# Spectral FFN on one Trainium2 core: low halves of the inverse-transform rows by TensorE and ScalarE from the third tile on, and another order of VectorE's spectral steps

## The chip, the cores and the metric

The kernel runs on one core of one Trainium2 chip. The metric is the device time of one execution in microseconds (us), the lower the better. The engines are TensorE (PE; its weight loads are PEld), VectorE (DVE), ScalarE (ACT), GpSimd (POOL) and SyncE (SP), each with its own instruction stream in program order; they meet through semaphores.

## What is computed

The reference has two parts in a row. The first is a spectral layer over x of shape 4 x 3008 x 256:

```
X  = rfft(x, axis=1)
Yr = Xr @ w_r - Xi @ w_i + b_r ;  Yi = Xr @ w_i + Xi @ w_r + b_i
Yr, Yi = sign(Y) * max(|Y| - 0.01, 0)
y  = irfft(Yr + i Yi, n=3008, axis=1)
```

The second is a feed-forward layer over all 12032 rows of y: h = y @ w_in (256 to 2048), g = (a0 + a1 h + a2 h^2 + a3 h^3) / (1 + |b0||h| + |b1| h^2 + 1e-6), out = g @ w_out (2048 to 256).

## The kernel before

The transform is factored as 3008 = 47 x 64. Step 1 (`step_s1`, 64 of them) transforms along one factor; its result goes to DRAM (`spec1`). Steps 2, 3 and 4 (`step_s2`, `step_s3`, `step_s4`, 96 of each: 24 in each of four batches) do the other factor, the mix with w_r and w_i with the threshold, and the inverse of that factor; the result goes to DRAM (`spec2`). Step 5 (`step_s5`) is the last part of the inverse and gives the rows of the feed-forward layer, transposed.

The feed-forward layer runs over 26 tiles (numbered from 0) of 470 rows (the last has 282). Each tile has 8 slots, so there are 208 slots; a slot handles 256 of the 2048 hidden columns. In a slot q the engines do, for a full tile:

- PE: `group_f2_hi(q-3)`, 8 matmuls; `group_f2_lo(q-3)`, 4 matmuls; `group_f1(q+2)`, 12 matmuls in float16; then spectral steps that fall into the slot, in the order 4, 3, 2, 1, 5 (lines 648 to 700).
- ACT: evacuations of steps 2, 1 and 5, then `group(q+1)` (three activations, den, sq, num, with the `below` of step 3 ahead of num), the store buffer o_sb once in a tile, a reciprocal root (L846), a square (L849), and the evacuation of step 4 (L750).
- DVE: L1087 and L1090 of slot q, `multiplied(q-2)` (L1067), `rounded(q-1)` (L1062), `remainder(q-2)` (L1073), and spectral steps between them: `lower_x` (L945, L948), `soft` (L954), `measure_x`, `measure`, `coefficients`, and `split_lo` (L1022).
- POOL: g_lo of group q-3 (L1148), which needs `remainder`, then a DMA that adds sq into den for group q+1 (L1140).

Step 2 is done in slots 0, 2, 4 and so on up to 138, without 94, 112 and 130; its step 3 comes one slot later and its step 4 three slots later. Step 1 is in slots 0 to 30 and 40 to 70, even ones. Step 5 of tile t is done in halves in slots 8(t-1)+1 and 8(t-1)+3 (`S5_AT`), so halves of tiles 2 to 18 are in slots 9 and 11, 17 and 19, up to 137 and 139. The steps 2, 4 and 5 share one PSUM bank, d0; 1 and 3 share d1. The waits that keep the shared bank in order are on the counts e4, e2l, e5l and k_top.

Every row tile is kept as two float16 parts, yt_hi and yt_lo, and `group_f1` multiplies both. There are two ways in which yt_lo is made:

- Tiles below 19: ACT evacuates the half of step 5 with the tile's scale into yt_hi (L762), and DVE's `split_lo` reads the bank again and writes bank x scale - yt_hi to yt_lo (L1022).
- Tiles from 19 on (`LATE_TILES`): step 5 uses a matrix that has the scale in it (`c5_scaled`, two of them, written by DVE at L1104 in slot 142). ACT copies the bank into yt_hi (L759) in the slot after; PE then adds -yt_hi to the bank with one matmul (`rest_of_s5`, L538) at the end of that slot; ACT copies the bank to yt_lo (L768) at the start of the slot after that.

`measure_x` is in slots 34 and 76, and `measure` with `coefficients` in slots 40, 88 and 142 (one set of scales for each combination of batches in a tile, seven in all; the first is made ahead of slot 0).

Of the kernel before, what the change touches and what calls it, by code (L numbers as in the profile page):

```python
# [19 lines left out]
ROWS = NJ * N2P  # L20
# [144 lines left out]
LATE_TILES = range(ENTRY[-1], NT)  # L165
# [19 lines left out]
def spectral_ffn(nc, x, c1, c5, fwd, inv, w_r, w_i, bias, w_in, w_out, coef_a, coef_b, out):  # L185
    with ExitStack() as ctx:
# [38 lines left out]
        c5_scaled = several("c5_scaled", 2, ROWS, PC)  # L225
# [69 lines left out]
        def scaled_c5(t):  # L295
            return c5_scaled[set_of(t) - set_of(LATE_TILES[0])]

# [158 lines left out]
        def _(pe):  # L456
# [64 lines left out]
            def step_s5(idx, bank):  # L521
                t, half = divmod(idx, KH)
                later = t in LATE_TILES
                pe.wait_ge(s_zp[t % 2], zp_count[t])
                if later:
                    pe.wait_ge(k_c5, set_of(t) - set_of(LATE_TILES[0]) + 1)
# [126 lines left out]
            for q in range(NS + 2):  # L653
# [6 lines left out]
                if q == NS + 1:  # L660
                    group_f2_lo(NS - 2)
                    group_f2_lo(NS - 1)
                if q + 2 < NS:
                    group_f1(q + 2)
# [34 lines left out]
                if q - 1 in S5_AT and S5_AT[q - 1] // KH in LATE_TILES:  # L699
                    rest_of_s5(S5_AT[q - 1], d0[:, :])  # L700

        @block.scalar
        def _(act):
# [49 lines left out]
            def evacuate_s5(idx, bank):  # L753
# [4 lines left out]
                if t in LATE_TILES:  # L758
# [6 lines left out]
            def evacuate_rest(idx, bank):  # L765
                t, half = divmod(idx, KH)
                act.wait_ge(e5r, idx - KH * LATE_TILES[0] + 1)
                act.activation(yt_lo[t % 2][:, half, 0:tile_cols(t)], bank[:, 0:tile_cols(t)], ACT.Copy).then_inc(e5l, 1)  # L768

            def group(q, c=None):  # L770
# [9 lines left out]
                if c is not None:  # L780
                    below(c, d1)
                act.activation(ring(num, q), h, ACT.Identity, bias=scales(q // SLOTS, 4),  # L782
                               scale=scales(q // SLOTS, 5)).then_inc(n_num, 1)

# [33 lines left out]
            for q in range(NS + 2):  # L818
# [11 lines left out]
                if q - 2 in S5_AT and S5_AT[q - 2] // KH in LATE_TILES:  # L830
                    evacuate_rest(S5_AT[q - 2], d0[:, :])
                if 1 <= q < NS - 1:
                    group(q + 1, S2_AT.get(q - 2))
# [22 lines left out]
        def _(dve):  # L856
# [149 lines left out]

            def weight_lo(i):
# [24 lines left out]
            for u in range(1, PRE + 1):  # L1032
# [16 lines left out]
                if u == K2 + 2:  # L1049
                    measure(0, (d0, d1)[(u - 1) % 2])  # L1050
                    coefficients(0)
                if u == PRE - 1:
# [30 lines left out]
            for q in range(NS + 2):  # L1083
# [8 lines left out]
                if q == 0:  # L1092
                    lower_x(PRE, d0[:, :])
                if q - 1 in S2_AT and q >= 2:
                    lower_x(S2_AT[q - 1], d0[:, :])
                if q - 1 in Y_AT:
                    n = Y_AT.index(q - 1)
                    measure(n, d0)
                    for i in range(len(SETS)):
                        if SETS[i][-1] == n:  # L1100
                            coefficients(i)
                        if SETS[i][-1] == n == B - 1:
                            dve.wait_ge(s_ff, 16)
                            dve.tensor_scalar(c5_scaled[i - set_of(LATE_TILES[0])][:, :], c5_sb[:, :],  # L1104
                                              coef[0:ROWS, i, 0:1], None, ALU.mult).then_inc(k_c5, 1)
                if 0 <= q - 2 < NS and late(q - 2):
                    multiplied(q - 2)
                if 0 <= q - 1 < NS:
# [3 lines left out]
                if q - 1 in S5_AT and S5_AT[q - 1] // KH not in LATE_TILES:  # L1112
# [66 lines left out]
```

## Time and profile before

| | us |
|---|---|
| median of 3 runs (lowest, highest) | 1448.93 (1446.75, 1450.62) |
| the profiled execution | 1448.17 |
| its span, first to last instruction | 1445.9 |
| PE busy | 1393.1 (96%) |
| DVE busy | 1324.2 (92%) |
| ACT busy | 1252.1 (87%) |
| POOL busy | 630.4 (44%) |

The granted clock of TensorE is 0.99 of full over the span. Around the span lie 2.3 us. Busy time counts neighbours that overlap in the pipeline once, and matmul ends are modelled, so a PE that is busy without a gap is seen better from the starts of its instructions than from their lengths. The slots run from 128 us (start of DVE's slot 0) to the end.

### The profile page before, as it was taken

The numbers are of one execution on the slowest core, as the hardware profiler recorded it, in microseconds if no ns is written. First come the engines' busy times: TensorE is split into PE (matmuls) and PEld (weight loads), VectorE is DVE, ScalarE is ACT, GpSimd is POOL, SyncE is SP. The second block draws the span as 40 slices with busy tenths as digits, with TensorE's granted clock in tenths as the row PEclk, the third lists the DMA queues.
The fourth block names the chain that finished last, engine by engine and source line by source line (L and its number), as shares of the span: only waits on it lengthen the run. The fifth ranks groups of instructions, "written<-read, shape, count | busy, mean of one in ns | idle before, by whom it ended". The sixth has DMA issues, their size and how long they took to land.

```text
span 1445.9 us, 21576 instructions
## 1 busy us (share of the span) xinstructions
PE 1393.1 (96%) x7498; PEld 972.8 (67%) x7498; DVE 1324.2 (92%) x1650; ACT 1252.1 (87%) x1657; POOL 630.4 (44%) x417
## 2 busy tenths in 40 slices
PE   7998999999999999999999999999989999999987
PEld 2876766667667676776766676776766666666666
DVE  5676989989999889899999999999999999999998
ACT  3577989988989989889879988988988999999986
POOL 0000444444444444444445445544545555555554
PEclk8999999999999999999999999999999999999999
DMA  8885665666556655555555545555545555555443
GB/s 257 265 258 137 151 152 136 143 144 137 108 124 150 142 119 134 136 114 118 110 120 114 126 108 123 124 113 111 114 105 108 107 94 110 118 108 110 86 97 70
DMA packets 97913, 188.07 MB, mean 130 GB/s; under 512 B 11216, under 2 KB 57744, under 8 KB 97808
## 3 DMA queue, kind: packets, MB, share of 16 engines
q0 software_dynamic: 29952, 98.58, 36.8%
q1 hardware_dynamic: 67856, 88.12, 20.7%
q8 instruction: 62, 1.02, 0.3%
q14 instruction: 43, 0.35, 0.1%
HBM read 50.60 MB, written 37.49 MB: 61 GB/s over the span
## 4 chain that ended last, share of the span: by engine, by line
PE 52%; DVE 20%; ACT 16%; issue 8%; DMA 2%; POOL 2%; SPq 0%; ACTq 0%; DVEq 0%; POOLq 0%
PE h_ps L552 18%; PE o_ps L582 7%; PE o_ps L567 6%; PE o_ps L569 6%; DVE num L1073 4%; DVE den L1067 4%; DVE g_hi L1062 4%; DVE num L1087 4%; PE d L529 3%; ACT sq L779 3%; ACT den L776 3%; ACT num L782 3%; ACT sq L846 3%; PE d L493 2%; POOL g_lo L1148 2%
## 5 line engine op out<-in xcount | busy, mean ns | idle before, releaser
L1148 POOL TENSOR_TENSOR g_lo<-num,sq 128x940 fp32r<-128x940 f32 (+1 forms) x205 | 453.1, 2210 | 153.2 <-DVE num L1073 153.1
L1140 POOL DMA_DIRECT2D den<-sq x208 | 182.5, 877 | 649.6 <-ACT sq L779 345.4
L567 PE MATMUL o_ps<-g_hi,wout_hi 128*128 128x470 f32 (+1 forms) x832 | 342.0, 412 | 1.0 <-DVE g_hi L1062 1.0
L569 PE MATMUL o_ps<-g_hi,wout_lo 128*128 128x470 f32 (+1 forms) x832 | 310.3, 374 | 0.0
L552 PE MATMUL h_ps<-yt_hi,win_hi 128*128 128x470 f16 (+1 forms) x832 | 302.2, 363 | 3.7 <-DVE num L1090 3.7
L552 PE MATMUL h_ps<-yt_hi,win_lo 128*128 128x470 f16 (+1 forms) x832 | 300.1, 361 | 0.0
L552 PE MATMUL h_ps<-yt_lo,win_hi 128*128 128x470 f16 (+1 forms) x832 | 300.0, 361 | 0.0
L1090 DVE SCALAR_TENSOR_TENSOR num<-num,coef,h_ps 128x940 f32<-128x940 f32 (+1 forms) x208 | 245.2, 1179 | 7.4
L1073 DVE SCALAR_TENSOR_TENSOR num<-num,a_sb,den 128x940 f32<-128x940 f32 (+1 forms) x208 | 244.6, 1176 | 0.1
L1062 DVE SCALAR_TENSOR_TENSOR g_hi<-num,a_sb,sq 128x940 fp32r<-128x940 f32 (+1 forms) x208 | 244.5, 1175 | 0.0
L779 ACT ACTIVATE sq<-h_ps,coef 128x940 f32<-128x940 f32 (+1 forms) x208 | 214.6, 1032 | 32.1 <-POOL g_lo L1148 31.9
L582 PE MATMUL o_ps<-g_lo,wout_hi 128*128 128x470 f32 (+1 forms) x832 | 216.0, 382 | 25.8 <-POOL g_lo L1148 24.9
L1087 DVE TENSOR_TENSOR num<-h_ps,num 128x940 f32<-128x940 f32 (+1 forms) x208 | 231.7, 1114 | 9.9 <-ACT num L782 9.6
L1067 DVE SCALAR_TENSOR_TENSOR den<-den,g_hi 128x940 f32<-128x940 f32 (+1 forms) x208 | 238.9, 1148 | 0.1
L782 ACT ACTIVATE num<-h_ps,coef 128x940 f32<-128x940 f32 (+1 forms) x208 | 234.2, 1126 | 0.0
L846 ACT ACTIVATE sq<-den,qone 128x940 f32<-128x940 f32 (+1 forms) x208 | 223.7, 1075 | 3.4 <-DMA den<-sq 3.4
L776 ACT ACTIVATE den<-h_ps,coef 128x940 f32<-128x940 f32 (+1 forms) x208 | 213.0, 1024 | 6.5 <-DVE num L1073 4.3
L849 ACT ACTIVATE sq<-sq 128x940 f32<-128x940 f32 (+1 forms) x208 | 203.2, 977 | 6.6
L582 PEld LDWEIGHTS o_ps<-g_lo,wout_hi 128*128 128x128 f32 x832 | 151.4, 190 | 64.0 <-POOL g_lo L1148 46.1
L567 PEld LDWEIGHTS o_ps<-g_hi,wout_hi 128*128 128x128 f32 x832 | 157.8, 190 | 31.0 <-issue 8.3
L569 PEld LDWEIGHTS o_ps<-g_hi,wout_lo 128*128 128x128 f32 x832 | 158.0, 190 | 23.4 <-issue 7.5
L552 PEld LDWEIGHTS h_ps<-yt_hi,win_hi 128*128 128x128 f16 x832 | 81.3, 98 | 113.9 <-issue 48.7
(161 smaller groups left out, 1576.8 us busy)
## 6 DMA issues: line engine op xcount, KB each, us to landing
den<-sq POOLq DMA_DIRECT2D x200, 470.0 KB, 4.4
spec<-s1w SPq DMA_DIRECT2D x64, 192.0 KB, 2.7
z_in<-spec SPq DMA_DIRECT2D x96, 128.0 KB, 2.5
spec<-s_out SPq DMA_DIRECT2D x96, 128.0 KB, 1.9
xw<-in_x SPq DMA_DIRECT2D x31, 384.0 KB, 4.7
out_t<-o_sb SPq DMA_DIRECT2D x25, 470.0 KB, 4.0
zp_in<-spec SPq DMA_DIRECT2D x22, 480.0 KB, 5.3
inv_in<-in_inv SPq DMA_DIRECT2D x96, 64.0 KB, 2.2
```

What stands on the lines that cost most here:

```text
L552: mm = pe.matmul(h_ps[q % 2][:, j, 0:cols(q)], w[:, h, f * P:(f + 1) * P], y[t % 2][:, h, 0:cols(q)], start=i == 0, stop=i == len(terms) - 1)
L567: pe.matmul(o_ps[:, h, 0:w], wout_hi[:, f, h * P:(h + 1) * P], g_hi[q % 3][:, j, 0:w], start=f == 0, stop=False)
L569: mm = pe.matmul(o_ps[:, h, 0:w], wout_lo[:, f, h * P:(h + 1) * P], g_hi[q % 3][:, j, 0:w], start=False, stop=False)
L582: mm = pe.matmul(o_ps[:, h, 0:w], wout_hi[:, f, h * P:(h + 1) * P], g_lo[q % 2][:, j, 0:w], start=False, stop=f == FB - 1)
L779: act.activation(ring(sq, q), h, ACT.Square, scale=scales(q // SLOTS, 3)).then_inc(n_sq, 1)
L782: act.activation(ring(num, q), h, ACT.Identity, bias=scales(q // SLOTS, 4), scale=scales(q // SLOTS, 5)).then_inc(n_num, 1)
L846: act.activation(ring(sq, q), ring(den, q), ACT.Abs_reciprocal_sqrt, bias=qone[:, 0:1]).then_inc(n_rs, 1)
L1062: dve.scalar_tensor_tensor(out=g_hi[r % 3][:, :, 0:w], in0=ring(num, r), scalar=a_sb[:, 0:1], in1=ring(sq, r), op0=ALU.add, op1=ALU.mult). ...
L1067: dve.scalar_tensor_tensor(out=ring(den, r), in0=ring(den, r), scalar=1.0 + 1e-6, in1=g_hi[r % 3][:, :, 0:cols(r)].bitcast(F32), op0=ALU.a ...
L1073: dve.scalar_tensor_tensor(out=ring(num, r), in0=ring(num, r), scalar=a_sb[:, 0:1], in1=ring(den, r), op0=ALU.add, op1=ALU.subtract).then_ ...
L1087: dve.tensor_tensor(top, h, top, ALU.mult).then_inc(n_n2, 1)
L1148: pool.tensor_tensor(g_lo[r % 2][:, :, 0:cols(r)], ring(num, r), ring(sq, r), ALU.mult).then_inc(n_g, 1)
```

## The change

Four things change.

1. `LATE_TILES` (19 to 25) becomes `PE_TILES` (2 to 25). `c5_scaled` has seven buffers, one for each set, and DVE writes the one that belongs to a set right behind that set's `coefficients`.
2. PE issues `rest_of_s5` in the same slot, but behind `group_f2_lo(q-3)` and ahead of `group_f1(q+2)`, no longer at the slot's end.
3. ACT copies the bank to yt_lo (`evacuate_rest`) in that same slot, behind the num activation of `group(q+1)`, no longer at the start of the next slot.
4. On DVE `lower_x` stands behind `multiplied(q-2)`, no longer ahead of `measure`; `remainder(q-2)` stands ahead of `soft` and `measure_x`, no longer behind them.

```diff
-LATE_TILES = range(ENTRY[-1], NT)
+PE_TILES = range(2, NT)
...
-        c5_scaled = several("c5_scaled", 2, ROWS, PC)
+        c5_scaled = several("c5_scaled", len(SETS), ROWS, PC)
...
+                if q - 1 in S5_AT and S5_AT[q - 1] // KH in PE_TILES:
+                    rest_of_s5(S5_AT[q - 1], d0[:, :])
                 if q + 2 < NS:
                     group_f1(q + 2)
...
                 if q in S5_AT:
                     step_s5(S5_AT[q], d0[:, :])
-                if q - 1 in S5_AT and S5_AT[q - 1] // KH in LATE_TILES:
-                    rest_of_s5(S5_AT[q - 1], d0[:, :])
...
                 act.activation(ring(num, q), h, ACT.Identity, bias=scales(q // SLOTS, 4),
                                scale=scales(q // SLOTS, 5)).then_inc(n_num, 1)
+                if rest is not None:
+                    evacuate_rest(rest, d0[:, :])
...
-                if q - 2 in S5_AT and S5_AT[q - 2] // KH in LATE_TILES:
-                    evacuate_rest(S5_AT[q - 2], d0[:, :])
                 if 1 <= q < NS - 1:
-                    group(q + 1, S2_AT.get(q - 2))
+                    group(q + 1, S2_AT.get(q - 2), S5_AT[q - 1] if S5_AT.get(q - 1, 0) // KH in PE_TILES else None)
...
+            def scaled_matrix(i):
+                dve.wait_ge(s_ff, 16)
+                dve.tensor_scalar(c5_scaled[i][:, :], c5_sb[:, :], coef[0:ROWS, i, 0:1], None, ALU.mult).then_inc(k_c5, 1)
...
-                if q == 0:
-                    lower_x(PRE, d0[:, :])
-                if q - 1 in S2_AT and q >= 2:
-                    lower_x(S2_AT[q - 1], d0[:, :])
                 if q - 1 in Y_AT:
                     n = Y_AT.index(q - 1)
                     measure(n, d0)
                     for i in range(len(SETS)):
                         if SETS[i][-1] == n:
                             coefficients(i)
-                        if SETS[i][-1] == n == B - 1:
-                            dve.wait_ge(s_ff, 16)
-                            dve.tensor_scalar(c5_scaled[i - set_of(LATE_TILES[0])][:, :], c5_sb[:, :],
-                                              coef[0:ROWS, i, 0:1], None, ALU.mult).then_inc(k_c5, 1)
+                            scaled_matrix(i)
                 if 0 <= q - 2 < NS and late(q - 2):
                     multiplied(q - 2)
+                if q == 0:
+                    lower_x(PRE, d0[:, :])
+                if q - 1 in S2_AT and q >= 2:
+                    lower_x(S2_AT[q - 1], d0[:, :])
                 if 0 <= q - 1 < NS:
                     rounded(q - 1)
                 if 1 <= q <= KH:
                     split_lo(KH + q - 1, o_ps[:, q - 1, :])
-                if q - 1 in S5_AT and S5_AT[q - 1] // KH not in LATE_TILES:
+                if q - 1 in S5_AT and S5_AT[q - 1] // KH not in PE_TILES:
                     split_lo(S5_AT[q - 1], d0[:, :])
+                if 0 <= q - 2 < NS and late(q - 2):
+                    remainder(q - 2)
+                    if on_vector(q - 2):
+                        lower(q - 2)
                 if q - 2 in S2_AT:
                     soft(S2_AT[q - 2], d1)
...
-                if 0 <= q - 2 < NS and late(q - 2):
-                    remainder(q - 2)
-                    if on_vector(q - 2):
-                        lower(q - 2)
```

## Rows read from the trace of the kernel before

**Rows 1.** The page, part 1: busy time, share, instructions of each engine.

```profile
PE 1393.1 (96%) x7498; PEld 972.8 (67%) x7498; DVE 1324.2 (92%) x1650; ACT 1252.1 (87%) x1657; POOL 630.4 (44%) x417
```

**Rows 2.** Busy time by stretch (start:end, length, then each engine's).

```profile
247.71:262.57 14.86, 14.38 (x82) 10.11 (x80) 11.76 (x15) 13.45 (x19) 5.58 (x4) 1.00 0.42 90
262.57:303.12 40.55, 40.55 (x218) 28.53 (x219) 38.30 (x45) 37.00 (x52) 19.02 (x13) 1.00 0.72 159
357.70:372.65 14.95, 13.71 (x80) 9.86 (x79) 13.11 (x25) 12.56 (x16) 5.25 (x5) 1.00 0.41 85
945.50:959.28 13.78, 13.57 (x79) 9.67 (x77) 12.29 (x16) 12.38 (x16) 5.67 (x5) 1.00 0.39 82
1150.56:1195.21 44.65, 43.42 (x215) 28.93 (x214) 44.31 (x41) 41.99 (x46) 24.76 (x16) 1.00 0.54 109
```

**Rows 3.** Waits of the whole span: waiter, releaser, us, times, longest.

```profile
PEld d L529 <- ACT s_out L750: 11.1, 16, 1.7
```

**Rows 4.** Timeline, slots 18 and 19: start, length, instruction, idle before it.

```profile
247.71 1.25 PE L529 MATMUL d<-c_sb,zp_in 96*128 96x94 f32 x10
249.00 0.65 ACT L762 ACTIVATE yt_hi<-d,coef 128x470 f16<-128x470 f32 x1 [2.03 <-PE d L529]
...
251.85 1.15 ACT L782 ACTIVATE num<-h_ps,coef 128x940 f32<-128x940 f32 x1
...
253.78 0.61 PE L469 MATMUL d<-fwd_sb,z_in 128*128 128x128 f32 x4
...
262.06 0.46 ACT L750 ACTIVATE s_out<-d,x_inv 128x256 f32<-128x256 f32 x1
262.57 1.35 PE L529 MATMUL d<-c_sb,zp_in 96*128 96x94 f32 x10 [0.48 <-ACT s_out L750]
```

**Rows 5.** Instruction groups by shape: count, busy us, mean ns, idle before.

```profile
L1022 DVE SCALAR_TENSOR_TENSOR yt_lo<-d,coef,yt_hi 128x470 f16<-128x470 f32 x34 | 23.8, 701 | 2.3 <-ACT yt_hi L762 2.3
L1104 DVE TENSOR_SCALAR c_scaled<-c_sb,coef 96x94 f32<-96x94 f32 x2 | 0.5, 268 | 0.1
```

**Rows 6.** Timeline of ACT in slots 154 and 155, a late tile.

```profile
1191.22 0.56 ACT L759 ACTIVATE yt_hi<-d 128x470 f16<-128x470 f32 x1 [0.61 <-PE d L529]
...
1197.42 0.54 ACT L768 ACTIVATE yt_lo<-d 128x470 f16<-128x470 f32 x1
1197.86 1.04 ACT L776 ACTIVATE den<-h_ps,coef 128x940 f32<-128x940 f32 x1
```

**Rows 7.** Timeline of PE's weight loads around the late tile's extra matmul.

```profile
1195.82 0.10 PEld L538 LDWEIGHTS d<-yt_hi,minus_one 128*128 128x128 f16 x1
1196.02 0.19 PEld L567 LDWEIGHTS o_ps<-g_hi,wout_hi 128*128 128x128 f32 x1
```

**Rows 8.** The chain that ended last: start, length, what; one group_f1.

```profile
149.00 2.40 PE h_ps L552 x12
```

**Rows 9.** Timeline, slot 34, and PE behind it.

```profile
362.14 0.88 POOL L1140 DMA_DIRECT2D den<-sq  x1 [4.41 <-PE o_ps L582]
...
363.90 1.20 DVE L1073 SCALAR_TENSOR_TENSOR num<-num,a_sb,den 128x940 f32<-128x940 f32 x1
...
367.44 1.13 PE L582 MATMUL o_ps<-g_lo,wout_hi 128*128 128x470 f32 x4 [1.24 <-POOL g_lo L1148]
```

**Rows 10.** Timeline, slots 84, 88 and 142, and PE behind slot 76.

```profile
657.52 1.13 PE L582 MATMUL o_ps<-g_lo,wout_hi 128*128 128x470 f32 x4 [1.26 <-POOL g_lo L1148]
...
705.20 1.15 ACT L782 ACTIVATE num<-h_ps,coef 128x940 f32<-128x940 f32 x1
705.36 0.42 DVE L954 SCALAR_TENSOR_TENSOR ythr<-d,neg 128x256 f32<-128x256 f32 x1 [0.61 <-ACT neg L739]
...
706.82 1.13 DVE L1087 TENSOR_TENSOR num<-h_ps,num 128x940 f32<-128x940 f32 x1
...
736.62 1.12 PE L582 MATMUL o_ps<-g_lo,wout_hi 128*128 128x470 f32 x4 [2.26 <-POOL g_lo L1148]
...
1084.76 1.93 PE L582 MATMUL o_ps<-g_lo,wout_hi 128*128 128x470 f32 x4 [3.54 <-POOL g_lo L1148]
```

More of the change, by code:

```diff
@@ L295, in scaled_c5 @@
         def scaled_c5(t):
-            return c5_scaled[set_of(t) - set_of(LATE_TILES[0])]
+            return c5_scaled[set_of(t)]
         def cols(q):
@@ L522, in step_s5 @@
                 t, half = divmod(idx, KH)
-                later = t in LATE_TILES
+                later = t in PE_TILES
                 pe.wait_ge(s_zp[t % 2], zp_count[t])
                 if later:
-                    pe.wait_ge(k_c5, set_of(t) - set_of(LATE_TILES[0]) + 1)
+                    pe.wait_ge(k_c5, set_of(t) + 1)
                 matrix = scaled_c5(t) if later else c5_sb
@@ L757, in evacuate_s5 @@
                     act.wait_ge(f1, (t - 1) * SLOTS)
-                if t in LATE_TILES:
+                if t in PE_TILES:
                     act.activation(yt_hi[t % 2][:, half, 0:tile_cols(t)], bank[:, 0:tile_cols(t)], ACT.Copy).then_inc(e5, 1)
@@ L766, in evacuate_rest, with group @@
                 t, half = divmod(idx, KH)
-                act.wait_ge(e5r, idx - KH * LATE_TILES[0] + 1)
+                act.wait_ge(e5r, idx - KH * PE_TILES[0] + 1)
                 act.activation(yt_lo[t % 2][:, half, 0:tile_cols(t)], bank[:, 0:tile_cols(t)], ACT.Copy).then_inc(e5l, 1)
-            def group(q, c=None):
+            def group(q, c=None, rest=None):
                 h = h_ps[q % 2][:, :, 0:cols(q)]
@@ L1051, in _ @@
                     coefficients(0)
+                    scaled_matrix(0)
                 if u == PRE - 1:
```

## The prediction

> **What bounds the kernel now.** I read the page's shares first. PE is busy for 96% of the span, DVE 92%, ACT 87% [rows 1]: three engines are near full, so shares alone don't tell what a microsecond on each is worth. The view by stretch does. While spectral steps run (slots 3 to 141, tiles 0 to 17), cut a tile's 8 slots at the two halves of step 5. From the second half to the next tile's first, PE is busy for 40.55 of 40.55 us while DVE works 38.30 and ACT 37.00 [rows 2]: PE sets the pace. Between the two halves it isn't quite so: 14.86 us, PE 14.38, and the stretch ends with PE waiting for ACT's evacuation of step 4 [rows 2, 4]. The timeline of ACT there has no gap: released by step 5 at 249.00, it runs through to 262.52, and step 5's other half starts at 262.57 [rows 4]. So this stretch is a loop through ACT's queue. The same wait stands in the list of waits 16 times [rows 3]; I count it in all 17 tiles but two. The exceptions are slot 35, where PE is late for another reason (below), and slot 115, which has no step 4; the sixteenth is the first half in slot 113. From slot 142 on, DVE is the bound: 44.31 busy of 44.65 us, PE 43.42 [rows 2].
>
> So VectorE, which the change relieves, is the bound in the last third only, where nothing is taken from it.
>
> **Part 1: split_lo leaves DVE.** 34 instructions of 0.70 us, 23.8 us in all [rows 5]. By the stretches above they lie beside PE's or ACT's work: worth nothing by themselves, but for the places in part 4.
>
> **Part 2: 34 more matmuls on PE.** In a late tile the same matmul's weight load starts at 1195.82 and the next one's at 1196.02, so it takes 0.20 us of PE's queue [rows 7]; 12 float16 matmuls of group_f1 take 2.40, again 0.20 each [rows 8]. The matmul now stands between float32 and float16 ones, which no row shows: bounds 0.10 (the transition partly hides it) and 0.30; I take 0.20, the spacing of its own kind. Its wait is over in time: yt_hi is done about 1.9 us after step 5 began (249.00 + 0.65 against 247.71) [rows 4], while PE still has the rest of step 5 and 12 matmuls of group_f2 in between, over 2.4 us at the spacing just named. Queued behind it are group_f1 and steps 4 to 1.
>
> The Trainium skill, "TensorE: Matmul & The Clock Gate", section "Back-to-back issue gap", gives a sustained 131 ns for a matmul of 512 columns in a stream of weight loads and matmuls. The trace differs, 0.20 us at 470 columns [rows 8]; by the page's figure part 2 would be about 4.5 us in place of 6.8, before anything is hidden, an estimate.
>
> **Part 3: 34 more copies on ACT.** One takes 0.54 us, but the next instruction starts 0.44 after it [rows 6]. The copy to yt_hi becomes one without a scale operand, 0.56 instead of 0.65 [rows 4, 6], 0.09 less. Net 0.35 in each slot that has one. The copy stands behind num, so DVE's L1087 isn't delayed; o_sb, the root and the square are, and with them the end of the ACT loop.
>
> Who waits for it: step 2 in the same slot, by the count e5l, since the bank is shared. num ends at 253.0 now (251.85 + 1.15), in future 0.09 earlier; the copy behind it ends by 253.45, while PE reaches step 2 at 253.78, in future 0.20 later [rows 4]. Cover about 0.5 us. If that cover were gone, each 0.1 us beyond would cost 34 x 0.1 = 3.4 us.
>
> The Trainium skill, "ScalarE: Activation LUTs", section "Rules for kernel authors", says to use VectorE, not ScalarE, for simple arithmetic; it speaks against this move. For this operation the trace has DVE at 0.70 and ACT at 0.54 [rows 5, 6]: per instruction it differs from the rule. By the rule the copy would take 0.70 or more, 0.16 x 15 = 2.4 us on top of the sum, an estimate.
>
> **Part 4: the order on DVE.** remainder goes ahead of soft and measure_x. Where that counts:
> - Slot 34: remainder starts at 363.90, behind the soft's wait and nine small instructions; PE then waits 1.24 us for the g_lo behind it, released by POOL [rows 9], and has taken some 0.16 more in the matmul before, 1.40 in all. With the new order remainder is some 3 us earlier, and POOL can start when its DMA ends, at 363.02 [rows 9], so 2.1 us before 365.1, where remainder ends now. The wait goes whole. Slot 76 is alike, 1.26 us [rows 10], 1.42 in all.
> - Slots 84 to 88: DVE runs without a gap from slot 84, where it has a wait of 0.61 and the split_lo, up to the coefficients in slot 88, behind which PE waits 2.26 us [rows 10]. With both gone, what is late next is ACT's num: 705.20 + 1.15 = 706.35, less 0.09, against L1087 at 706.82 now [rows 10]. Gain about 0.5; the two new c5_scaled cost 2 x 0.18 of queue (0.27 us long) [rows 5], which soft's move behind remainder (0.35) takes back. The same 0.5 in front of slot 142, behind which PE waits 3.54 and which leads into the stage that DVE bounds [rows 10]. In slot 40 step 1 waits for soft, which now comes later: +0.1.
> - lower_x behind multiplied: a slot's group_f1 (2.40 us) [rows 8] stands ahead of its reader, step 3, on PE. Nothing.
> - Elsewhere PE doesn't wait for DVE or POOL, so nothing.
>
> **The sum**, per stretch.
> - First to second half, 15 tiles bound by ACT: +0.35 each (PE's 0.20 fits under it), 5.25. Slot 115's: +0.20. Slots 33 to 35: the stretch is 14.95 now; the stall goes, and next is the ACT loop, 13.78 where there is no step 1 [rows 2], plus 0.35, 14.13: -0.8. Together +4.65.
> - Second half to next tile, 17: 11 at +0.20 are 2.2; slot 40 +0.1; slot 76 -1.42 + 0.20 = -1.2; slot 88 -0.5; slot 142 -0.5; two around the slots that have no step 2 (94, 112), where PE loses a few tenths to POOL, -0.5 together, an estimate from those slots' pace. Together -0.4.
> - From slot 142 on: the copy only moves within ACT's queue, DVE's work is the same: 0. Ahead of slot 3 one c5_scaled more (0.27 us) under a wait for ACT: 0.
>
> Sum +4.2 us on the profiled execution's 1448.2, 1452.4. That one is 0.8 below the median of the runs; from the median it would be 1453.1. I say 1452.8.
>
> **The rivals.**
> - A, the gains don't come: POOL or ACT holds slots 34, 76, 88, 142 as DVE did. For: POOL's DMA stands in the way in slot 34. Against: it ends in time. 17 x 0.35 + 17 x 0.20 = +9.4: 1458.
> - B, slower by one mechanism: step 2 waits for the yt_lo copy on the shared bank. Place: slots 10, 12, 18, 20 and so on. It decides once ACT's copy ends over 0.5 us later than I place it. At 0.2 beyond, 34 x 0.2 = 6.8 on top of 4.2: 1460. For: ACT's queue there is without gaps. Against: both sides hang on the same step 5, so the cover is the same in each tile.
> - C, the matmul is cheap (0.10) and PE's small losses to DVE and POOL go with DVE's relief: 11 x 0.10 less and some 2 us from 8 tiles without step 1: 1449.5.
> - D, faster: the bound in tiles 9 to 17 is really DVE, which works 38.30 of 40.55 us in such a stretch [rows 2]. Then 1.2 us of split_lo goes in each of 9 tiles, 10.8, against 2 of additions: 1440. Against: PE has no idle time in that stretch [rows 2].
> - E, the change doesn't do what it says (split_lo stays, the matmul goes elsewhere): the code leaves no room for it.
>
> **How the numbers follow.** Forecast (1450.5 to 1455) 0.50, C 0.22, A 0.12, B 0.07, D 0.09. 0.3% of 1448.9 is 4.3 us, about what a measurement can tell from no change: 1444.6 to 1453.3. Of the forecast's chance 0.28 lies below 1453.3, so same = 0.28 + 0.22 = 0.50; faster is D, 0.09; slower 0.22 + 0.12 + 0.07 = 0.41. The range reaches from 1446.5, below C (the added matmuls at 0.10 throughout, and all waits of PE for POOL gone), to 1458, A; outside are D and B. Its ends follow the two unknown costs: 34 matmuls at 0.10 or 0.30, and the copy at 0.44 or 0.54.
>
> **What would show it.** In the profile after: L1022 down to 4 instructions; DVE's busy time down by 20 or more us and the span not; the stretch from step 5 to step 5 at 15.2 us with step 1 and 14.1 without, ended by ACT's s_out; the other stretch at 40.75 with PE busy throughout; no PE wait for POOL behind slots 34 and 76; DVE idle where it worked. The prediction is wrong if the first stretch doesn't grow (then ACT's queue wasn't the loop), if the other shrinks (then PE wasn't the bound), or if step 2 starts late behind L768.

## The result, and the profile after

The changed kernel takes 1453.35 us (median; 1450.94 to 1455.58), the kernel before 1448.39 (1446.71 to 1450.62) on the same chip. The ratio is 1.0033 with a 95% interval of 1.0023 to 1.0042: slower by about 5 us. I had said 1452.8; by my own bounds for no change, 0.3%, the time lies just above the edge. The profiled execution took 1452.47 with a span of 1450.5 against 1445.9 (4.5 more; both are rounded).

First the page's busy times. They answer to [rows 1]:

```profile
PE 1394.7 (96%) x7532; PEld 976.5 (67%) x7532; DVE 1315.8 (91%) x1621; ACT 1262.1 (87%) x1691; POOL 631.9 (44%) x417
```

PE and ACT have their 34 instructions more, DVE has 29 fewer. DVE's busy time fell by 8.4 us only. The groups of instructions by shape say why:

```profile
L768 ACT ACTIVATE yt_lo<-d 128x470 f16<-128x470 f32 x46 | 26.8, 583 | 0.0
L1009 DVE TENSOR_SCALAR c_scaled<-c_sb,coef 96x94 f32<-96x94 f32 x7 | 1.9, 267 | 0.2
L1072 DVE SCALAR_TENSOR_TENSOR den<-den,g_hi 128x940 f32<-128x940 f32 x200 | 237.5, 1188 | 0.0
L1150 POOL TENSOR_TENSOR g_lo<-num,sq 128x940 fp32r<-128x940 f32 x200 | 462.9, 2315 | 89.4 <-DVE num L1078 89.2
```

23.8 us of split_lo went [rows 5] and 1.4 of c5_scaled came. But `multiplied` (L1072) now has a mean of 1188 ns and 237.5 us in all, where L1067 had 231.5 before, and POOL's g_lo has 2315 ns where L1148 had 2227: the same work shows as longer, on both engines. For POOL that goes with what stands in front: its g_lo lasts 2.16 to 2.23 us wherever POOL stood idle before it (172 of 200 before, 117 now), and 2.4 to 2.5 in most cases where it follows POOL's DMA instruction at once (13 times before, 79 now). Why, no row shows. POOL's waits for `remainder` fell from 153.1 us to 89.2, most of which shortened nothing.

`multiplied` is held by POOL. Two lines of slot 18:

```profile
245.58 2.50 POOL L1150 TENSOR_TENSOR g_lo<-num,sq 128x940 fp32r<-128x940 f32 x1
247.76 1.32 DVE L1072 SCALAR_TENSOR_TENSOR den<-den,g_hi 128x940 f32<-128x940 f32 x1
```

g_lo ends at 248.08, `multiplied` 1.00 later. So it is each time: of the 200 full ones 150 take 1.13 us, and none of them starts more than 0.14 ahead of g_lo's end; the other 50 start 0.29 to 1.04 ahead of it and end 1.00 after it (0.99 to 1.01). In the kernel before there are 26 of those. Over 1.13 they make up 11.5 us in place of 5.5, which is the 6.0.

The span is read better by stretch. The same columns as in [rows 2], same stretches in the changed kernel, in time order:

```profile
248.58:263.80 15.22, 14.57 (x83) 10.20 (x81) 11.78 (x15) 13.81 (x20) 5.99 (x4) 1.00 0.41 89
263.80:304.46 40.66, 40.66 (x218) 28.60 (x219) 37.72 (x43) 37.30 (x53) 18.74 (x13) 1.00 0.69 157
359.65:373.90 14.25, 13.77 (x81) 9.95 (x80) 12.18 (x22) 12.74 (x17) 4.27 (x4) 1.00 0.37 78
949.84:963.98 14.14, 13.70 (x80) 9.85 (x78) 12.72 (x16) 12.74 (x17) 6.44 (x5) 1.00 0.39 80
```

From first to second half of step 5 it is 15.22 for 14.86, and 14.14 for 13.78: +0.36 each. From second half to the next tile it is 40.66; from start of step 5 to start of step 5 it had been 40.49 (the row in [rows 2] ends 0.06 later), so +0.17.

Cutting the whole span at the starts of step 5 and adding up (us, after less before):

| stretches | foretold | measured |
|---|---|---|
| first to second half, 15 bound by ACT | +5.25 | +5.40 |
| the one from slot 113 | +0.20 | +0.17 |
| slots 33 to 35 | -0.8 | -0.70 |
| second half to next tile, 11 of 17 | +2.2 | +1.75 |
| from slot 35 (slot 40) | +0.1 | +0.28 |
| from slot 75 (slot 76) | -1.2 | -0.17 |
| from slot 83 (slot 88) | -0.5 | -0.50 |
| from slots 91 and 107 | -0.5 | -0.75 |
| from slot 139 (slot 142) | -0.5 | -1.75 |
| from slot 145 to slot 195 | 0 | +0.07 |
| before slot 9 and behind slot 195 | 0 | +0.72 |
| sum | +4.2 | +4.5 |

Two terms missed by over 1 us, in opposite directions, from slot 75 and from slot 139. The experiments below take these up, and the loop through ScalarE.

The timeline of slot 18 answers to [rows 4]: PE's matmul, ACT's copy, what follows each, and the end of the loop.

```profile
252.26 0.37 PE L538 MATMUL d<-yt_hi,minus_one 128*128 128x470 f16 x1
252.47 0.36 PE L552 MATMUL h_ps<-yt_hi,win_hi 128*128 128x470 f16 x1
...
253.65 0.59 ACT L768 ACTIVATE yt_lo<-d 128x470 f16<-128x470 f32 x1
...
254.09 0.99 ACT L839 ACTIVATE o_sb<-o_ps 128x940 f32<-128x940 f32 x1
...
254.85 0.61 PE L469 MATMUL d<-fwd_sb,z_in 128*128 128x128 f32 x4
...
263.29 0.46 ACT L750 ACTIVATE s_out<-d,x_inv 128x256 f32<-128x256 f32 x1
263.80 1.35 PE L529 MATMUL d<-c_scaled,zp_in 96*128 96x94 f32 x10 [0.65 <-ACT s_out L750]
```

The matmul holds PE's queue for 0.21 (252.26 to 252.47), the copy holds ACT's for 0.44 (253.65 to 254.09). The copy ends at 254.24 and step 2 starts at 254.85: a distance of 0.61 us is left.

### The profile page after: what moved, and what is told of

It is laid out like the page before. It is cut to its first block, busy times and chain, and to the rows that moved or that the text cites. A ratio compares the mean times of both kernels' runs of the same rounds, so it can differ in the third digit from the quotient of the medians.

```text
span 1450.5 us, 21719 instructions
## 1 busy us (share of the span) xinstructions
PE 1394.7 (96%) x7532; PEld 976.5 (67%) x7532; DVE 1315.8 (91%) x1621; ACT 1262.1 (87%) x1691; POOL 631.9 (44%) x417
## 4 chain that ended last, share of the span: by engine, by line
PE 54%; DVE 19%; ACT 16%; issue 8%; POOL 1%; DMA 1%; ACTq 0%; SPq 0%; DVEq 0%; POOLq 0%
PE h_ps L552 18%; PE o_ps L582 7%; PE o_ps L567 6%; PE o_ps L569 6%; DVE den L1072 4%; DVE num L1078 4%; DVE num L1092 4%; DVE g_hi L1067 4%; PE d L529 3%; ACT den L776 3%; ACT sq L779 3%; ACT sq L846 2%; PE d L493 2%; ACT num L782 2%; PE o_ps L463 2%
## 5 line engine op out<-in xcount | busy, mean ns | idle before, releaser
L1150 POOL TENSOR_TENSOR g_lo<-num,sq 128x940 fp32r<-128x940 f32 (+1 forms) x205 | 470.8, 2297 | 89.4 <-DVE num L1078 89.2
L552 PE MATMUL h_ps<-yt_hi,win_hi 128*128 128x470 f16 (+1 forms) x832 | 300.5, 361 | 4.6 <-DVE num L1095 4.6
L552 PE MATMUL h_ps<-yt_lo,win_hi 128*128 128x470 f16 (+1 forms) x832 | 298.9, 359 | 0.0
L552 PE MATMUL h_ps<-yt_hi,win_lo 128*128 128x470 f16 (+1 forms) x832 | 298.9, 359 | 0.0
L1092 DVE TENSOR_TENSOR num<-h_ps,num 128x940 f32<-128x940 f32 (+1 forms) x208 | 232.1, 1116 | 38.6 <-ACT num L782 37.9
L1095 DVE SCALAR_TENSOR_TENSOR num<-num,coef,h_ps 128x940 f32<-128x940 f32 (+1 forms) x208 | 245.2, 1179 | 7.4
L1072 DVE SCALAR_TENSOR_TENSOR den<-den,g_hi 128x940 f32<-128x940 f32 (+1 forms) x208 | 245.1, 1178 | 0.0
L1067 DVE SCALAR_TENSOR_TENSOR g_hi<-num,a_sb,sq 128x940 fp32r<-128x940 f32 (+1 forms) x208 | 244.2, 1174 | 0.0
L582 PE MATMUL o_ps<-g_lo,wout_hi 128*128 128x470 f32 (+1 forms) x832 | 215.0, 381 | 21.2 <-POOL g_lo L1150 20.9
L582 PEld LDWEIGHTS o_ps<-g_lo,wout_hi 128*128 128x128 f32 x832 | 153.4, 190 | 55.6 <-POOL g_lo L1150 36.8
L552 PEld LDWEIGHTS h_ps<-yt_hi,win_hi 128*128 128x128 f16 x832 | 81.3, 98 | 103.2 <-issue 35.9
```

What stands on the lines that cost most here:

```text
L552: mm = pe.matmul(h_ps[q % 2][:, j, 0:cols(q)], w[:, h, f * P:(f + 1) * P], y[t % 2][:, h, 0:cols(q)], start=i == 0, stop=i == len(terms) - 1)
L582: mm = pe.matmul(o_ps[:, h, 0:w], wout_hi[:, f, h * P:(h + 1) * P], g_lo[q % 2][:, j, 0:w], start=False, stop=f == FB - 1)
L1067: dve.scalar_tensor_tensor(out=g_hi[r % 3][:, :, 0:w], in0=ring(num, r), scalar=a_sb[:, 0:1], in1=ring(sq, r), op0=ALU.add, op1=ALU.mult). ...
L1072: dve.scalar_tensor_tensor(out=ring(den, r), in0=ring(den, r), scalar=1.0 + 1e-6, in1=g_hi[r % 3][:, :, 0:cols(r)].bitcast(F32), op0=ALU.a ...
L1092: dve.tensor_tensor(top, h, top, ALU.mult).then_inc(n_n2, 1)
L1150: pool.tensor_tensor(g_lo[r % 2][:, :, 0:cols(r)], ring(num, r), ring(sq, r), ALU.mult).then_inc(n_g, 1)
```

## The experiments

In all twelve, differences of stretches come from the start of step 5 in one kernel's trace against the other's; medians and intervals are of kernels run together on one chip. Where there is one execution only, I say so and go by stretches; two kernels at the end that are equal but for slot 40 agree within 0.04 us in every stretch that neither slot 40 nor the clock behind slot 142 touches.

### The order alone, and the move alone

The kernel before with part 4 of the change only:

```diff
+                if 0 <= q - 2 < NS and late(q - 2):
+                    remainder(q - 2)
...
                 if q - 2 in S2_AT:
                     soft(S2_AT[q - 2], d1)
...
-                if 0 <= q - 2 < NS and late(q - 2):
-                    remainder(q - 2)
```

> The kernel before with the new VectorE order alone (part 4); split_lo, the scaled matrices and the late tiles as before. Theory (TensorE and a loop through ScalarE's queue set the pace of the spectral stage; the order removes single TensorE waits): between the halves of step 5 14.86 us with step 1 and 13.78 without, as before; slots 33 to 35 from 14.95 to 13.8; slot 75 to 81 from 39.40 to between 38.0 (all of the wait gone) and 39.0 (if picks is held up by GpSimd's g_lo as in the changed kernel); slots 83 to 89 and 139 to 145 0.5 to 1.8 less each. Sum -4 to -6 us: about 1443.5. Rival (the order is worth nothing by itself, the gains in those slots came from split_lo's going): under 1 us, 1448. Rival (VectorE sets the pace of the spectral stage): 1448 as well, since VectorE's work stays the same.

Measured: 1446.62 us, ratio 0.9984 (0.9975 to 0.9993). Less than expected: slot 33's stretch -0.60, slot 75's -0.07, those from 83, 91, 107 and 139 -0.78, -0.42, -0.41 and -0.38, but the one from slot 35 +2.08.

The changed kernel with DVE's old order:

```diff
                 if q - 2 in S2_AT:
                     soft(S2_AT[q - 2], d1)
...
+                if 0 <= q - 2 < NS and late(q - 2):
+                    remainder(q - 2)
```

> The changed kernel with VectorE's steps back in the old order (parts 1 to 3 alone). Theory: stretches between the halves 15.22 and 14.14 us as in the changed kernel, the others +0.17 each; the TensorE waits behind slots 34 and 76 are back; slots 83 to 89 about as before or +0.3; sum +7 to +9 us against before: about 1456.5, ratio 1.0055. Rival (split_lo's removal is what gave the gains, not the order): like the changed kernel, +4 to +5, 1453. Rival (VectorE is the bound, so 23.8 us less of its work help): below 1448.

Measured: 1457.41, ratio 1.0064 (1.0051 to 1.0076). First stretches +0.37 (slot 9's +0.47), the 11 second ones +0.11 to +0.20 but for slot 115's +0.03. Parts 1 to 3 cost 9 us, the order gives 4 of them back in the changed kernel but 2 on the kernel before. By stretch the order gives nearly the same in both: in the changed kernel against this one -0.61 from slot 33, -0.10 from 75, -0.86, -0.52, -0.24 and -0.62 from 83, 91, 107 and 139. What is missing on the kernel before is the +2.08 from slot 35, which comes up again below.

The count of held `multiplied` follows the order too: 50 with the new order alone, 19 in this kernel. They cost the pace nothing that the stretches show, but they are why VectorE's busy time fell so little.

### Why slot 76 gained nothing

In the changed kernel PE waits behind slot 76 no longer for POOL, as foretold. This is the timeline there (DVE, POOL, PE):

```profile
656.75 2.49 POOL L1150 TENSOR_TENSOR g_lo<-num,sq 128x940 fp32r<-128x940 f32 x1
657.51 0.15 DVE L938 TENSOR_SCALAR x_lam<-x_out 128x1 f32<-128x1 f32 x1
657.58 1.75 DVE L939 TENSOR_SCALAR picks<-pick,x_out 128x128 bf16<-128x128 f32 x1
659.37 1.14 DVE L1092 TENSOR_TENSOR num<-h_ps,num 128x940 f32<-128x940 f32 x1
...
661.79 0.37 PE L552 MATMUL h_ps<-yt_hi,win_hi 128*128 128x470 f16 x1 [0.44 <-DVE num L1095]
```

The `picks` instruction of `measure_x` takes 1.75 us. In the kernel before the same instruction took 0.28:

```profile
653.68 0.28 DVE L939 TENSOR_SCALAR picks<-pick,x_out 128x128 bf16<-128x128 f32 x1
```

It ends at 659.33, and POOL's g_lo ends at 659.24. Before, g_lo came behind measure_x, since it needs `remainder`; with remainder first, the two meet. Behind picks stand L1092 and L1095, and PE's group_f1 waits for L1095. Against a gain of 1.42 on PE's wait for POOL, DVE pays 1.47. The Trainium skill, "SBUF — State Buffer", section "SBUF: two separate sides", has a rule for it: VectorE and GpSimd share a pair of ports under an exclusive lock, wanted by VectorE operations in a 2-port mode or (against a GpSimd operation that reads SBUF) with two operands in SBUF, and whoever starts first keeps it for the whole instruction. The trace agrees with the course of it, and for `multiplied`, which has two operands in SBUF, with the condition too; in which mode `picks` runs no row shows. Not everything is held: the five 128x1 `TENSOR_SCALAR` of `measure_x` that stand in front of picks run beside the same g_lo at their usual 0.15 to 0.20.

The test takes that one instruction off DVE, in slots 34 and 76:

```diff
+                for n in (2, 3):
+                    if q == X_AT[n] + 1:
+                        act.wait_ge(k_x, X_STEPS * (n + 1) - 1)
+                        act.activation(picks[n][:, :], pick[:, :], ACT.Identity, scale=x_out[:, n:n + 1]).then_inc(k_x, 1)
```

> The changed kernel with one small instruction of measure_x (picks, 128x128) done by ScalarE in slots 34 and 76 instead of VectorE. In the changed kernel it takes 1.75 us there and ends 0.09 us after GpSimd's g_lo, against 0.28 before. Theory (it is held up until GpSimd's tensor instruction ends, and that delays VectorE and so TensorE's group_f1): the ScalarE form takes about 0.35 us, VectorE's L1092 comes 1 us or more earlier, TensorE's wait of 0.44 for VectorE behind slot 76 is gone, slot 75 to 81 from 39.23 to about 38.2. Rival (picks was slow for its own position behind x_out, and TensorE's loss is elsewhere): slot 75 to 81 stays within 0.2 of 39.23.

Measured (one execution): 1450.42. The stretch from slot 75 is 1.35 below the kernel before, where the changed kernel was 0.17 below. The same place in its timeline:

```profile
655.96 2.50 POOL L1155 TENSOR_TENSOR g_lo<-num,sq 128x940 fp32r<-128x940 f32 x1
656.73 0.15 DVE L942 TENSOR_SCALAR x_lam<-x_out 128x1 f32<-128x1 f32 x1
656.80 1.13 DVE L1097 TENSOR_TENSOR num<-h_ps,num 128x940 f32<-128x940 f32 x1
```

L1097 starts 0.84 after g_lo and takes its usual 1.13 beside it; one of its operands is in PSUM. So POOL doesn't hold DVE as such, but certain instructions, and the missing 1.2 us are explained. In slots 33 to 35, though, this kernel is 0.26 worse than the changed one. There the changed kernel's PE has waited 0.48 for L1095, and now it waits 0.73 for ACT's s_out: ACT's loop got one instruction more.

### The slow clock behind slot 142, and slots 40 and 88

PE waits there for 3.35 to 3.61 us in the four kernels below, and the stretch still differs by up to 1.75. The clock column of the view by stretch, for the 10 us from the end of that wait (kernel before; changed; order alone; old order; in this order):

```profile
1084.76:1094.76 10.00, 10.00 (x36) 5.85 (x37) 9.55 (x9) 7.86 (x8) 4.38 (x4) 0.73 0.27 51
```

```profile
1090.06:1100.06 10.00, 10.00 (x42) 6.27 (x43) 9.93 (x10) 9.05 (x10) 5.08 (x4) 0.85 0.39 73
```

```profile
1083.33:1093.33 10.00, 10.00 (x36) 5.80 (x37) 9.49 (x9) 7.81 (x8) 4.31 (x4) 0.72 0.27 51
```

```profile
1093.78:1103.78 10.00, 10.00 (x41) 6.16 (x42) 9.93 (x10) 8.87 (x9) 5.08 (x4) 0.84 0.37 69
```

A mean of 0.73 and one of 0.85 differ by 1.2 us of work in 10. That is the surplus. The changed kernel (0.85) has -1.75, the old order (0.84) -1.12, order alone (0.72) -0.38: less 1.2 where the clock was higher, the order gives 0.4 to 0.55, and the old order nothing, as foretold. Why the slow time is shorter in some executions I can't say. It isn't the order: two nearly equal kernels at the end of this section have 0.72 and 0.83. Whether parts 1 to 3 have to do with it stays open: all nine traces of kernels that have them show 0.83 to 0.85, four of the five without them 0.72 to 0.74, and only the fifth 0.83.

The same explains slot 40 of the order-alone kernel, where step 1 waits for `soft`. The 10 us behind the wait, and the wait:

```profile
404.87:414.87 10.00, 10.00 (x48) 7.35 (x49) 9.89 (x11) 5.91 (x7) 4.87 (x3) 0.83 0.30 61
```

```profile
404.87 1.07 PE L463 MATMUL d<-xw,c_sb 96*96 96x512 f32 x2 [2.10 <-issue]
```

By the clock column 1.7 us of the stretch's +2.08 are the clock's. In the changed kernel the same wait is 1.61 and the clock stays at 1.00. Without the slow clock this execution's span would have been some 3.2 below the kernel before's, not 1.5.

Could `measure` and `coefficients` go behind `soft`, so that soft isn't late?

```diff
                 if q - 2 in S2_AT:
                     soft(S2_AT[q - 2], d1)
+                if q - 1 in Y_AT:
+                    n = Y_AT.index(q - 1)
+                    measure(n, d0)
...
```

> The changed kernel with measure, coefficients and the scaled matrices behind soft in slots 40, 88 and 142, instead of ahead of multiplied. Theory: TensorE's waits there go (1.6 us for step 1 in slot 40, 1.7 for g_lo in slot 88, 3.4 for g_lo in slot 142). Slots 35 to 41 from 41.08 to 39.4, slots 83 to 89 from 40.36 to 38.7, slots 139 to 145 from 37.04 to 36.5, since VectorE sets the pace from there and its work is the same; the granted clock stays at 1.00 through slot 142, where it is 0.5 now. About -4 us: 1449.5. Rival (coefficients are needed so soon that somebody else waits for them): the same time as the changed kernel.

Measured: 1455.83, ratio 1.0054 (1.0041 to 1.0067). My expectation missed: the waits for g_lo went, others came, and the stretch from slot 83 is 2.29 longer than in the changed kernel, that from 139 1.45 longer. Slot 88 in its timeline:

```profile
734.37 2.18 POOL L1150 TENSOR_TENSOR g_lo<-num,sq 128x940 fp32r<-128x940 f32 x1 [0.53 <-DVE num L1078]
...
735.19 1.38 DVE L993 TENSOR_TENSOR y_pair<-y_binade 128x1 f32<-128x1 f32 x1
...
741.76 0.37 PE L552 MATMUL h_ps<-yt_hi,win_hi 128*128 128x470 f16 x1 [2.38 <-DVE num L1095]
```

The chain of small instructions now stands in front of L1092, and it too meets g_lo: y_pair, of 128x1 elements, takes 1.38 us where it takes 0.16 in the changed kernel (731.66), and ends with g_lo. The wait moved from L582 to L552. Behind it the clock is at a mean of 0.83 for 10 us, 1.7 of the 2.29; the medians, which don't hang on one execution, still differ by 2.5 (taken on two chips; the ratios to the kernel before differ by 0.0021, 3 us). How little a wait's length says of the clock, slot 88 shows: PE waits 2.26 us for g_lo there in the kernel before and also in a kernel further down (step 4 earlier on the kernel before), and the 10 us behind it are

```profile
736.62:746.62 10.00, 10.00 (x59) 7.33 (x60) 9.36 (x13) 7.93 (x11) 3.50 (x3) 1.00 0.36 81
```

```profile
731.64:741.64 10.00, 10.00 (x51) 6.95 (x52) 8.95 (x10) 6.34 (x8) 3.06 (x2) 0.83 0.37 81
```

### Doubling the two terms of the move

A second matmul of zero weights next to the added one, which adds nothing to the result:

```diff
+                pe.matmul(bank[:, 0:w], no_weight[:, :], yt_hi[t % 2][:, half, 0:w],
+                          start=False, stop=True, skip_group_check=True)
```

> The changed kernel with a second matmul of the same shape with zero weights ahead of each extra matmul, so that the work on TensorE is doubled and the values stay. Theory: in the stretches between the halves, which ScalarE's loop sets, nothing (15.22 and 14.14 stay within 0.05); in the others, which TensorE sets, +0.20 each (40.66 to 40.86), nothing from slot 142 on. In all about 12 x 0.2 = +2.4 us. Rival (TensorE sets the first stretch too): +0.20 there as well, +5.5 in all. Rival (the matmul's cost is hidden or only a transition's): under 0.05 in every stretch.

Measured (one execution): first stretches +0.37 over the kernel before, as without it; second ones +0.31 to +0.39 (slot 115's +0.23), so 0.2 more. Slot 113's first stretch, where ACT's loop isn't the bound, also took 0.22 more. PE's 0.20 counts where PE is busy throughout, and is hidden where ACT's loop is longer.

A second copy on ACT, of 352 columns into a spare buffer:

```diff
+                act.activation(spare[:, 0:min(352, tile_cols(t))], bank[:, 0:min(352, tile_cols(t))], ACT.Copy).then_inc(k_spare, 1)
```

> The changed kernel with one more ScalarE copy (352 columns of the same bank into a spare tile) ahead of each copy to yt_lo. Its cost in ScalarE's queue is about 0.35 us. Theory: stretches between the halves +0.35 each (15.57 and 14.5), where TensorE sets the pace nothing (40.66 within 0.05) unless step 2 begins to wait for the later copy (cover 0.5 us, so just not), nothing from slot 142 on. About 15 x 0.35 = +5 us. Rival (ScalarE's queue has slack in the first stretch): under 0.1 there.

Measured (one execution): 1463.74. First stretches +0.35 more, the 11 second ones together +1.9, and +2.5 from slot 145 on, which I had not foreseen in that size: in the late tiles ACT has less slack than its share of 87% lets expect. Of the +1.9, 1.6 are in the single stretch from slot 131, and they are the clock's: PE has waited 1.57 us for ACT in front of it, and the 10 us behind are

```profile
1022.49:1032.49 10.00, 10.00 (x47) 7.67 (x48) 7.86 (x9) 7.67 (x11) 3.31 (x3) 0.83 0.75 183
```

which is 1.7 us lost. The other ten took 0.3 together, so a longer copy still costs the second stretches next to nothing.

### Is the cover of step 2 real?

The matmul behind group_f1, so that ACT's copy is later against step 2:

```diff
-                if q - 1 in S5_AT and S5_AT[q - 1] // KH in PE_TILES:
-                    rest_of_s5(S5_AT[q - 1], d0[:, :])
                 if q + 2 < NS:
                     group_f1(q + 2)
+                if q - 1 in S5_AT and S5_AT[q - 1] // KH in PE_TILES:
+                    rest_of_s5(S5_AT[q - 1], d0[:, :])
```

> The changed kernel with the extra matmul behind group_f1 instead of ahead of it, still ahead of step 2 in the same slot. Theory: ScalarE's copy then waits for the matmul by about 1.3 us and step 2 by about 0.8 us for the copy on the shared bank: the stretches between the halves about +1.3 (16.5 and 15.4), the others +0.8 (41.4 and 38.9), 15 to 30 us more in all, so 1470 to 1480. That is the price behind the 0.5 us of cover that the prediction counted. Rival (the order of the matmul and group_f1 doesn't matter because ScalarE has slack): within 1 us of the changed kernel.

Measured (one execution): 1512.94, far above what I had expected. Over the changed kernel it is +1.4 in each first stretch, +1.0 in each second one, +1.8 and +1.2 from slot 145 on. The late tiles, which I had left out, make 19 of the 60 us; for the rest my figures per stretch (1.3 and 0.8) were near, but 17 of each are 36 us, not the 15 to 30 that I wrote. In slot 18:

```profile
256.72 0.36 PE L538 MATMUL d<-yt_hi,minus_one 128*128 128x470 f16 x1
257.11 0.56 ACT L768 ACTIVATE yt_lo<-d 128x470 f16<-128x470 f32 x1 [1.27 <-PE d L538]
...
257.89 0.68 PE L469 MATMUL d<-fwd_sb,z_in 128*128 128x128 f32 x4 [0.81 <-issue]
```

ACT stands for 1.27 us, and PE for 0.81 until the copy has left the bank. PE starts 0.22 after the copy's end (257.67), so of the changed kernel's distance of 0.61 about 0.4 is cover. That fits the longer copy above: with 0.35 more in front, the copy ended at 255.96 and step 2 of slot 18 still came in time, at 256.23. This is rival B; the changed kernel avoids it by 0.4 us.

### ScalarE's loop

If the first stretches are a loop through ACT's queue with step 4's evacuation at its end, then moving that evacuation ahead of the square must shorten them. In the slots of second halves:

```diff
+                early = q - 3 in S2_AT and q in S5_AT and q - 2 in S5_AT
+                if early:
+                    evacuate_s4(S2_AT[q - 3], d0[:, :])
                 if q < NS:
                     act.wait_ge(n_rs, q + 1)
                     act.activation(ring(sq, q), ring(sq, q), ACT.Square).then_inc(n_rec, 1)
-                if q - 3 in S2_AT:
+                if q - 3 in S2_AT and not early:
                     evacuate_s4(S2_AT[q - 3], d0[:, :])
```

On the changed kernel:

> The changed kernel with ScalarE's evacuation of step 4 between the reciprocal root and the square in the slots of step 5's second half (11, 19, 27 and so on), instead of behind the square. Theory (the stretch between the halves is a loop through ScalarE's queue that ends with this evacuation): it ends 0.9 us earlier, TensorE then sets the stretch: 15.22 becomes 14.4 with step 1 and 14.14 becomes 13.5 without, the other stretches stay at 40.66 and 38.1; about -10 us in all, 1443. Rival (TensorE is what sets that stretch): within 0.1 per stretch, 1453. Rival (the later square holds VectorE's g_hi and hands the time back): first stretches shorter, second longer by as much.

Measured: 1439.98, ratio 0.9947 (0.9933 to 0.996), below both kernels and 3 us below what I had expected. The two kinds of first stretch:

```profile
247.50:261.90 14.40, 14.40 (x82) 10.30 (x81) 10.94 (x14) 13.08 (x20) 5.16 (x4) 1.00 0.37 82
939.98:953.51 13.53, 13.53 (x81) 9.94 (x79) 12.12 (x15) 12.21 (x17) 5.82 (x5) 1.00 0.35 75
```

PE is busy for all of 14.40 and 13.53 us. The loop is gone, and PE bounds there too. The second stretches gain 0.10 to 0.14 more; step 5 right behind its wait takes 1.35 in the timeline, and 1.25 where it needn't wait.

On the kernel before, with split_lo left on DVE:

> The kernel before, with ScalarE's evacuation of step 4 between root and square in the slots of second halves; nothing else. Theory (first stretches are a loop through ScalarE, and PE's own work is the floor below it): on the changed kernel this edit brought the first stretches to 14.40 and 13.54 us, where PE has no wait left; without the added matmul's 0.20 PE's floor here is 14.20 and 13.34. So 7 stretches x 0.66 and 7 x 0.44, one at 0.8: -8.5 us, about 1440. The second stretches unchanged. Rival (VectorE's work, split_lo included, stands right behind ScalarE's): the first stretches stay above 14.4 and 13.54, the time above 1443. If the theory holds, parts 1 to 3 of the change (a matmul and a copy for a split_lo) bring nothing even where ScalarE's loop is gone.

Measured: 1440.28, ratio 0.9945 (0.9933 to 0.9958), as expected; its profiled execution has the slow clock of slot 88 shown above, +1.56 in that stretch.

```profile
247.90:262.11 14.21, 14.21 (x81) 10.21 (x80) 11.10 (x14) 12.89 (x19) 4.93 (x4) 1.00 0.39 86
```

14.21 against 14.40: the difference is the added matmul. The relief of DVE isn't needed even here.

### The parts that help, together

The changed kernel with step 4 earlier and picks by ScalarE:

> The changed kernel with ScalarE's step 4 earlier, and the picks matrices of slots 34 and 76 written by ScalarE. Theory: the two gains are in different stretches and add: 1440.0 less 1.2 in the stretch from slot 75, 1438.6. Rival (ScalarE's extra instruction meets the moved evacuation): no better than 1440.

Measured: 1438.46, ratio 0.9936 (0.9924 to 0.9948); the stretch from slot 75 -1.37, as expected.

The kernel before with the new order, step 4 earlier and picks by ScalarE:

> The kernel before with the new VectorE order, step 4 earlier and picks by ScalarE; split_lo stays on VectorE for tiles up to 18. Theory: the order's -2, the loop's -8.5 and the picks' -1.3 add: 1436.8; the stretch from slot 35 keeps its +2.1, since step 1 of slot 40 waits for soft. Rival (parts 1 to 3 give VectorE the slack that the other gains need): 1440 or more, above the changed kernel with the same two edits.

Measured: 1431.89, ratio 0.9888 (0.9875 to 0.9902), the best of all and 5 us below what I had expected. Page and one first stretch of it:

```profile
PE 1383.5 (97%) x7498; PEld 973.2 (68%) x7498; DVE 1328.9 (93%) x1648; ACT 1249.7 (87%) x1659; POOL 632.0 (44%) x417
```

```profile
831.56:844.89 13.33, 13.33 (x80) 9.86 (x78) 12.45 (x16) 12.01 (x16) 5.77 (x5) 1.00 0.38 79
```

PE works 9.6 us less than in the kernel before (waits that end in a lower clock and the dearer step 5 are in that number), DVE 4.7 more, and from slot 9 up to slot 141 PE has only two waits over 0.3 us that come from DVE's work, 1.54 us for soft in slot 40 and 1.57 for the g_lo behind slot 88. By stretch against the kernel before: the 15 first ones -8.4, slots 33 to 35 -1.51, from slot 75 -1.52, from 83, 91, 107 and 139 -0.86, -0.54, -0.53 and -0.42. The largest part of what I missed, 2.1 of 5 us, is the stretch from slot 35: -0.03, not +2.1. Step 1 waits 1.54 there, and the clock doesn't fall behind it:

```profile
401.34:411.34 10.00, 10.00 (x57) 7.48 (x58) 9.89 (x11) 6.83 (x9) 4.89 (x3) 1.00 0.43 96
```

Another 0.9 is in slots 33 to 35, which I had counted at what order alone gave (-0.60), and 0.9 in the 15 first stretches (-8.4 for the -7.6 that the earlier step 4 alone gave; without step 1 13.33 for 13.42).

This kernel and the one before it differ by parts 1 to 3 alone. Without them it is 6.6 us faster, though ScalarE's loop and picks are mended in both.

The same with soft ahead of remainder in slot 40:

```diff
+                if q == 40:
+                    soft(S2_AT[q - 2], d1)
                 if 0 <= q - 2 < NS and late(q - 2):
                     remainder(q - 2)
```

> As the kernel with order, step 4 earlier and picks on the kernel before, but in slot 40 soft stands ahead of remainder, as it was. Theory: the +2.1 of the stretch from slot 35 came from step 1 waiting for soft behind remainder, and goes: 2 us below that kernel, 1434.8. Rival (it came from the lowered clock alone, or from lower_x's place): no difference.

Measured: 1432.42, ratio 0.9889 (0.9876 to 0.9902): no difference. The expectation missed. The stretch from slot 35 is 0.25 shorter than without it, no more: the +2.08 of order alone was mostly the clock's. These two kernels are equal but for slot 40, so what else differs between their executions is what one execution can differ by: step 5 of slot 9 starts at 191.75 in one and 192.76 in the other, and behind slot 142 the clock is

```profile
1069.21:1079.21 10.00, 10.00 (x35) 5.76 (x36) 9.42 (x9) 7.73 (x8) 4.25 (x4) 0.72 0.27 51
```

```profile
1069.94:1079.94 10.00, 10.00 (x41) 5.75 (x42) 9.93 (x10) 8.73 (x9) 5.07 (x4) 0.83 0.36 69
```

which makes 1.00 us in that stretch.

## Why the prediction was right

**What bounds.** Right, and the loop was shown by breaking it: step 4's evacuation ahead of one square took 0.5 to 1.0 us from each of the 15 first stretches of the changed kernel and left PE busy throughout. That VectorE's relief is worth nothing was right too: 1431.9 was reached with split_lo on DVE, 6.6 us below the same kernel with parts 1 to 3.

**Part 2**, 0.20 us per matmul: 0.21 in the timeline, 0.2 when doubled. The 11 stretches took +1.75, not 2.2, 0.16 each; the 0.04 between I can't place. The 131 ns of the Trainium skill ("TensorE: Matmul & The Clock Gate", "Back-to-back issue gap") aren't reached in this queue.

**Part 3**, the copy at 0.44, net 0.35: 0.44 and 0.36. The cover of step 2, said to be about 0.5, is 0.61 as I had counted it, and 0.4 when the 0.22 from the copy's end to PE's start is taken off. The estimate that I had drawn from the rule of the Trainium skill ("ScalarE: Activation LUTs", "Rules for kernel authors") had a first stretch grow by 0.51; it grew by 0.36. The move was still a loss, since VectorE's time was free and ScalarE's wasn't.

**Part 4** is where two terms of the sum were mis-sized, and they cancelled. That the sum came out within 0.3 us is luck. Slot 76 was put at -1.2 and gave -0.17: I had moved `remainder` ahead without asking what then runs beside the g_lo that it releases. Slot 34 has the same instruction held (1.76 us at 365.45). Its -0.8 was nearly met (-0.70), but not by the cause that I named: next late isn't ACT's evacuation but L1095, for which PE waits 0.48. Without the hold and the loop that stretch gives -1.51. Slot 88's -0.5 came, with PE's wait down from 2.26 to 1.67. Slot 142 was put at -0.5 and gave -1.75; about 1.2 of it is a shorter time at the lower clock, and whether that comes from the change is open. Without it the sum would have been +5.7.

**The tail and the start**, put at 0, gave +0.7. Kernels that are alike up to slot 9 differ by 1.0 us there, so nothing follows from it.

**What would show it.** The step "DVE's busy time down by 20 or more" failed, at 8.4. 23.8 went with split_lo; 1.4 came with c5_scaled, 3.0 with the two held picks, 6.0 with `multiplied`. That leaves 5.0. It is overlap: the durations of all DVE instructions, added up, fell by 14.1 us (1415.7 to 1401.6), the busy time, which counts overlapping neighbours once, by 8.4. An instruction that leaves takes less from the busy time than it lasts, by what it shared with its neighbours. `multiplied` is longer because the new order lets more of them start while POOL's g_lo still runs.

**Rivals.** A (gains don't come) was half right at slot 76, with DVE and not POOL as the one that holds; B is real at a distance of 0.4 us; C fell with the matmul's 0.21, D with every PE-bound stretch that didn't shrink.

## What to carry to other kernels

Before relieving a busy engine, cut the span where one step recurs and see which engine is busy for all of each stretch: here the fullest queue after PE's was on no path, while one square in front of an evacuation cost 0.5 us a tile in the mean of 15. When an instruction is moved ahead, look at what it releases and what will then run beside that; some instructions, short ones too, don't end before their neighbour does. And count a wait together with what the clock does behind it, but compare such stretches between kernels only at equal granted clock.

## What the hardware showed that I had not expected

- A VectorE instruction of 0.28 us (128x128, f32 to bf16) took 1.75 beside GpSimd's tensor_tensor, and one of 0.16 (128x1, two operands) 1.38; both ended within 0.1 us of GpSimd's instruction. One with an operand in PSUM kept its 1.13. `multiplied`, 128x940 with two operands in SBUF, was held 50 times and ended 1.00 after GpSimd's each time. It and the held 128x1 operation, which also has two operands in SBUF, agree with the rule of the Trainium skill named above; for the first one no row shows the condition.
- After a PE wait of about 3.5 us the granted clock was low for part of the next 10 us: means of 0.72 to 0.85. In the kernel before the group_f1 behind it took 4.04 us at a clock of 0.54, which is near the lower of its two levels (1.2 GHz), where it takes 2.40 at the full clock [rows 8]. After a wait of 2.26 it was 1.00 in one execution and 0.83 in another, after one of 2.10 0.83, after 1.54 and 1.61 1.00, but after one of 1.57 0.83. One such spell is 1.7 us, a third of what this change did.
